# An attention, expert and dense block in one program: routing inside the attention block, and expert tiles gathered row by row

## What is computed

```python
# 1: attention of 4 batches x 8 heads, 576 positions, head size 64
scores = scale * q_rot @ k_rot.T ;  attn = softmax(scores) ;  x = attn @ v      # -> [2304, 512]
# 2: one expert of eight for each token
logits = (x / (|x| + 1e-6)) @ (emb / (|emb| + 1e-6)).T / tau
e = argmax(logits) ;  gate = softmax(logits)[e]
y = gate * (relu(x @ w1[e]) @ w2[e])                                          # 512 -> 1024 -> 512
# 3: dense
h = y @ w_in ;  out = (h - tanh(h)) @ w_out                                   # 512 -> 2048 -> 512
```

## Time and profile before

| | us |
|---|---|
| median of 3 runs (lowest, highest) | 1116.12 (1115.24, 1118.18) |
| the profiled execution's own time | 1110.96 |
| its span in the trace | 1109.1 |
| PE busy / DVE / ACT / POOL | 985.1 / 595.5 / 582.4 / 415.7 |
| mean granted clock of TensorE | 0.964 |

### The profile page before, as it was taken

How to read it: one execution, slowest core, us unless ns; L and a number is a source line. 1 busy time by engine, 2 the same in 40 slices (tenths; PEclk the granted TensorE clock), 3 DMA queues, 4 the chain that set the end, 5 groups by cost and what they waited for, 6 DMA issues and landing times. The chain is left out here.

```text
span 1109.1 us, 18954 instructions
## 1 busy us (share of the span) xinstructions
PE 985.1 (89%) x5604; PEld 871.1 (79%) x5605; DVE 595.5 (54%) x1195; ACT 582.4 (53%) x1273; POOL 415.7 (37%) x246
## 2 busy tenths in 40 slices
PE   1899999999995039999999976999999999999996
PEld 1899899989984038888888855888989889899895
DVE  4677777777773731111111104777666666666764
ACT  1677777777772632222322214666565565655653
POOL 3998788887510428309948305000000000000000
PEclk9999999999998569999999997999999999999999
DMA  8777777767503455314433106111000000000001
GB/s 236 192 207 197 219 189 202 206 186 205 145 21 90 169 188 202 97 47 151 152 123 113 38 30 200 58 48 48 1 19 10 0 28 0 13 15 0 28 2 28
DMA packets 63077, 113.82 MB, mean 103 GB/s; under 512 B 20032, under 2 KB 24640, under 8 KB 61120
## 3 DMA queue, kind: packets, MB, share of 16 engines
q1 hardware_dynamic: 52352, 92.62, 29.0%
q10 hardware_dynamic: 7808, 11.31, 3.2%
q0 software_dynamic: 2880, 9.44, 2.5%
HBM read 60.58 MB, written 24.41 MB: 77 GB/s over the span
## 5 line engine op out<-in xcount | busy, mean ns | idle before, releaser
L1429 PE MATMUL hd_ps<-y_hi,w_hi 128*128 128x384 f32 x384 | 130.9, 341 | 7.8 <-DVE g_sb L1599 7.8
L1429 PE MATMUL hd_ps<-y_lo,w_hi 128*128 128x384 f32 x384 | 129.6, 338 | 0.0
L1429 PE MATMUL hd_ps<-y_hi,w_lo 128*128 128x384 f32 x384 | 129.3, 337 | 0.0
L1499 ACT ACTIVATE mag<-hd_ps 128x384 f32<-128x384 f32 x96 | 47.3, 493 | 152.2 <-PE hd_ps L1429 149.8
L617 DVE TENSOR_REDUCE neg_max<-ps 128x1 f32<-128x576 f32 x144 | 108.1, 751 | 31.4 <-PE ps L373 28.9
L633 DVE TENSOR_TENSOR pt_lo<-ps,pt_hi 128x512 fp32r<-128x512 f32 x144 | 99.2, 690 | 43.3 <-ACT pt_hi L538 41.7
L538 ACT ACTIVATE pt_hi<-ps 128x512 fp32r<-128x512 f32 x144 | 86.8, 604 | 58.9 <-PE ps L420 57.5
L1447 PE MATMUL o_ps<-w_hi,g_hi 128*128 128x512 f32 x288 | 115.0, 399 | 2.2 <-DVE g_lo L1608 2.2
L1447 PE MATMUL o_ps<-w_hi,g_lo 128*128 128x512 f32 x288 | 114.3, 397 | 0.0
L1608 DVE TENSOR_TENSOR g_lo<-g_sb,g_hi 128x384 fp32r<-128x384 f32 x96 | 53.5, 558 | 112.3 <-ACT g_hi L1514 112.3
L1447 PE MATMUL o_ps<-w_lo,g_hi 128*128 128x512 f32 x288 | 113.5, 394 | 0.0
(11 more groups left out here) (208 smaller groups left out, 2429.8 us busy)
## 6 DMA issues: line engine op xcount, KB each, us to landing
w_stage<-in_w SPq DMA_DIRECT2D x32, 512.0 KB, 3.6
raw_qk<-in_qk SPq DMA_DIRECT2D x14, 1152.0 KB, 6.1
k_hh<-qk_hi SPq DMA_DIRECT2D x64, 144.0 KB, 2.8
k_ll<-qk_lo SPq DMA_DIRECT2D x64, 144.0 KB, 2.9
sorted_rows<-zeros SPq DMA_DIRECT2D x28, 256.0 KB, 6.2
x_row<-sorted_rows ACTq DMA_DIRECT2D x20, 256.0 KB, 2.7
y_rows<-y_row ACTq DMA_DIRECT2D x20, 256.0 KB, 2.1
q_st<-qk_hi SPq DMA_DIRECT2D x32, 144.0 KB, 3.0
```

The lines of the kernel that those rows point to most:

```text
L1429: op = nc.tensor.matmul(hd_ps[f % 2][:, 0:G], w[:, c, cols], y[:, c, :], start=c == 0 and h == 0, stop=c == DC - 1 and h == 2)
```

## The change

**One block less.** `routing` is gone; its work stands at the end of each engine's part of `attention`. All buffers of attention are laid by hand (`spots`) over the place where the weights will be, so that the first weights can be split before the block ends.

**A normalised table, first thing.** The router table is squared, summed, square-rooted and inverted before the first rotation, and multiplied by 1/(norm tau) into `fold_sb`. The logits' shares then come out of the fold matmul ready.

**A gather in place of the scatter.** Token rows are stored in token order in `x_rows` (SP, plain DMAs, three of four batches during pair 12). From the slots a table of token numbers `gid` is made: `slot_hot` (which slot in a tile) times `tile_ids` (token number, for the tile it lies in), 18 matmuls with 50 columns. Tile t is then gathered by an indirect DMA with `gid[:, t]`. The first gather is issued in `attention`, seven at the start of `experts`, 17 after the first weight set split by POOL.

**Around it.** Three of the 18 square sums go into pair 14 on ACT, the other 15 behind the last pair. Slots and plan use scans and bit masks. `gate` is computed inside `experts`. The first half of the first expert's weights is rounded by ACT in `attention` (L832 there), its low half split in `experts`, and the tile 0 `up` does the products with the low weights last. PE's tile loop is written out: 15 tiles straight, 7 each under an If. The 28 clears of `sorted_rows` and two of three loads of the identity matrix are gone.

```diff
 def attention(...)                                     # tensor engine, behind the last fold
+            pe.wait_ge(hot_done, 1)
+            nc.tensor.matmul(total_ps, sums_r[:, 1, :], hot[:, 6:8 + E * T], start=True, stop=True).then_inc(counted, 1)
+            nc.tensor.matmul(rank_ps..., sums_r[:, 0, :], hot[:, 8:8 + E * T], start=True, stop=True).then_inc(ranked, 1)
+            for t in range(T):
+                if t % (T // 3) == 0:
+                    pe.wait_ge(slots_hot, t // (T // 3) + 1)
+                last = nc.tensor.matmul(id_ps, slot_hot[:, t, :], tile_ids[:, t, :, :]..., start=t == 0, stop=t == T - 1)
+            last.then_inc(ids_ready, 1)
...
 # vector engine, ahead of rope_first
+            dve.wait_ge(emb_in, 32)
+            nc.vector.tensor_tensor(emb_sq[:], emb_sb[:], emb_sb[:], ALU.mult).then_inc(emb_squared, 1)
+            dve.wait_ge(emb_summed, 1)
+            nc.vector.tensor_scalar(emb_n[:, 0, :], norm_ps, 1e-30, None, ALU.max).then_inc(emb_clamped, 1)
+            dve.wait_ge(emb_root, 1)
+            newton(chain, nc, emb_n[:, 2, :], emb_n[:, 1, :], emb_n[:, 0, :], emb_n[:, 3, :])
+            chain(nc.vector.tensor_scalar(emb_n[:, 4, :], emb_n[:, 2, :], inv_tau, None, ALU.mult))
             dve.wait_ge(tables_in, 32)
             rope_first(1, first_k_in, first_k_mult, first_k_done)
...
 # sync engine
-                if clears:
-                    for i in range(2):
-                        clear(sorted_dram, p * 2 - 2 + i)
+            body(PAIRS - 4, 0, more_raw=False)
+            for b in range(B - 1):
+                store_main(b, slice(0, D))
+            for t in range(T, MT):
+                sp.dma_start(y_dram[t * P:(t + 1) * P, :], zeros[:]).then_inc(zeroed, 16)
+            body(PAIRS - 3, 1, more_raw=False)
...
+            sp.wait_ge(x_done, PAIRS * 2)
+            pass_tail(PAIRS - 1, 1, "logits", last_logits)
+            store_main(B - 1, late)
+            pass_tail(PAIRS - 1, 1, "rows", last_in)
+            sp.wait_ge(first_set, 1)
+            for c in range(UP):
+                sp.dma_start(staged(stage, c), weight_chunk(a["w1"], a["w2"], expert, c)).then_inc(w_in0[c], 16)
...
 # gpsimd
-            pool.wait_ge(pos_done, 1)
-            for t in range(T):
-                pool.indirect_dma_start(sorted_dram, bass.IndirectOffsetOnAxis(pos_i[:, t:t + 1], 0),
-                                        x_all[:, t, :], None).then_inc(scattered, 16)
+            pool.wait_ge(gid_done, 1)
+            gather_x(nc, x_dram, rows, gid, 0).then_inc(first_x, 16)
...
 # experts: tensor and scalar engine
-            with pe.Fori(1, MT - 2) as t:
-                with pe.If(t < fourth + 2):
+            for t in range(1, T - 2):
+                tile(t)
+            for t in range(T - 2, MT - 2):
+                with pe.If(fourth > t - 2):
                     tile(t)
...
+            nc.scalar.activation(work[:], work[:], ACT.Exp).then_inc(exp_done, 1)
+            tile(0, start=True, split=True)
```

More of the change, by code:

```diff
@@ L68, in attention @@
         MAIN = FULL * P
[L70 to L88, removed]
@@ L490, in body @@
                         values(p, r, follow[i][1])
+            pe.wait_ge(sums_set, 1)
+            pe.wait_ge(emb_squared, 1)
+            for c in range(DC):
+                last = nc.tensor.matmul(norm_ps, sums[:, 1, :], emb_sq[:, c, :], start=c == 0, stop=c == DC - 1)
+            last.then_inc(emb_summed, 1)
             pe.wait_ge(cleared, 1)
@@ L598, in _ @@
+            act.wait_ge(last_in, 32)
+            square(T - 1)
+            act.wait_ge(first_set, 1)
+            slot = act.value_load(plan[0:1, SLOT, 0:1], min_val=0, max_val=1)
+            for c in range(UP):
+                act.wait_ge(w_in0[c], 16)
+                nc.scalar.activation(chunk_of(w_hi, slot, c), stage[:, c, :], ACT.Identity).then_inc(w_hi0, 1)
+            act.wait_ge(sq_done, T)
+            nc.scalar.activation(norm[:, 1, :], norm[:, 0, :], ACT.Sqrt, bias=least)
         @block.vector
@@ L766, in routing @@
-        logits = sb("logits", [P, T, E])
-        work = sb("work", [P, T, E])
-        onehot = sb("onehot", [P, T, E])
-        col = sb("col", [P, 4, T])
-        scan = [sb(f"scan{r}", [P, PAD + T, E]) for r in range(2)]
-        base = sb("base", [P, T, E])
-        over = sb("over", [P, E, T])
-        escan = [sb(f"escan{r}", [P, EPAD + E]) for r in range(2)]
-        start = sb("start", [P, E])
-        first_row = sb("first_row", [P, E])
-        parity = sb("parity", [P, E])
-        has = sb("has", [P, 4, E])
@@ L1115, in _, with gather @@
                     split_set(before, slot)
+            def gather(t):
+                if t >= HELD:
+                    pool.wait_ge(xt_ready, t - HELD + 1)
+                gather_x(nc, x_dram, rows, gid, t).then_inc(x_in[t], 16)
+            nc.gpsimd.memset(one[:], 1.0).then_inc(one_set, 1)
+            for t in range(1, AHEAD):
+                gather(t)
+            pool.wait_ge(one_set, 1)
+            pool.wait_ge(w_split, CHUNKS)
+            last = pool.value_load(plan[0:1, LAST, 0:1], min_val=0, max_val=E - 1)
+            with pool.Fori(0, 1) as before:
+                next_set(before)
+            for t in range(AHEAD, MT):
+                gather(t)
+            with pool.Fori(1, E - 1) as before:
+                next_set(before)
             split_set(last, 0)
+            for t in range(1, MT):
+                pool.wait_ge(x_in[t], 16)
         @block.tensor
```

804 lines of the change are left out of this document (451 added, 353 removed).

## The result

| | before | changed kernel |
|---|---|---|
| median of the runs, us | 1116.5 (4 runs, 1115.24 to 1118.18) | 1106.51 (4 runs, 1106.22 to 1106.9) |
| profiled execution, us | 1110.96 | 1106.22 |
| its span, us | 1109.1 | 1104.4 |
| granted clock | 0.964 | 0.965 |

The ratio is 0.991, with a 95% interval of 0.9893 to 0.9927: 10.0 us gained where 23 were forecast. 1106.5 lies 2.5 above the range. The profile of the kernel before is an execution 5.5 faster than the median of its timed runs, so the two spans differ by less than the medians do.

What follows compares the result with a forecast made beforehand. PE was taken as nearly full except for a hole at the routing block and another at the start. Terms +5.2 + 1.0 - 31.6 + 2.5 = -22.9, from 1116.12, gave 1093 us; range 1086 to 1104.

Steps and rivals of the forecast that it cites:

- start: Beginning of the kernel: the first rope waits behind the router table's norm, delaying PE's first matmul, +5.2 us.
- last pairs: End of attention: three square sums added to ACT in pair 14 delay the exp that PE needs, +1.0 us.
- hole: Routing between attention and experts, PE nearly idle: the new chain brings the experts' first transpose earlier, -31.6 us.
- first tiles: Start of the experts: the second half of the weights is split later, so `down(0)` comes later, +2.5 us.
- Dense keeps its order: Dense stage after the experts: its order is unchanged, so the sum has no term for it.
- rival (b): PE's written-out tile loop: five skips over tiles' code cost 4.5 us, giving 1098; chance 0.08.
- POOL's 17 gathers ... = 21.6 us: Experts, behind POOL's first weight set: gathers of 1.27 us each, 21.6 us, hidden by POOL's 43.3 us of idle time.
- Rival (e): Experts: gathers of 4.2 us each on POOL delay the second weight set by 33 us, giving 1126; chance 0.05.
- rival (d): Late attention: stores and clears ahead of SP's last stacking make pair 15 wait about 9 us, 1102; chance 0.06.
- rival (a): Routing: the index chain is dearer, 3.1 us for strided reads and about 2 for scans and int32, 1098; chance 0.16.
- the 5.2: Whole kernel: the median of the runs is 5.2 us above the profiled execution, 1110.96; the forecast starts from that median.

Runs made afterwards that it cites:

- e5: The changed kernel, unchanged, run again on a chip where the kernel before takes 1111.15 us: 1090.16 us, ratio 0.9809.
- e2: Changed kernel with only PE's seven conditional tiles in a run-time loop, VectorE copying their rows to one fixed place: 1083.69 us, ratio 0.9761.
- e4: The kernel before with only PE's tile loop written out, 15 tiles straight and 7 each under an If: 1119.56 us, ratio 1.0076.
- e14: Changed kernel with the 17 gathers split, eight behind the first weight set and nine behind the second: 1096.73 us, ratio 0.9825.
- e21: Changed kernel with all 24 gathers ahead of the first weight set, on a chip with stalls: 1105.84 us, ratio 0.9917.
- e6: Changed kernel with VectorE roping first and doing the table's norm behind `by_cos` and `by_sin`: 1092.8 us, ratio 0.9828.
- e9: Changed kernel with ScalarE's queue issuing the cosine and sine tables ahead of the expert table and tau: 1109.79 us.
- e10: Changed kernel with the cosine and sine tables first in ScalarE's queue and the ropes ahead of the norm on VectorE: 1106.16 us.
- e15: The kernel before, unchanged, run for its trace on a further chip: 1111.59 us, one execution.
- e11: Changed kernel with late tiles in a run-time loop (rows staged from tile 18 on), tables and ropes first, gates' exp early: 1098.21 us, ratio 0.9818.
- e12: Changed kernel with the exp of the gates, with its table load, moved ahead of `take_x(1)`: 1109.54 us.
- e20: Changed kernel with late tiles in a run-time loop, start reordered, exp before the first relu, gathers in two parts: 1087.08 us, ratio 0.9744.
- e1: Changed kernel with all PE tiles in a run-time loop, VectorE copying each tile's rows to one fixed place: 1084.89 us, ratio 0.9772.

## Why the prediction was wrong

On chip A 10.0 us were gained, 12.9 less than forecast. Of these, 16.4 are what the changed kernel loses between chip C and chip A (1090.16 and 1106.51), less 5.4 that the kernel before loses between them (1111.15 and 1116.5), and 1.9 are missing on chip C too. On a quiet chip the forecast was nearly right: 22.9 forecast, 21.0 measured by the medians (e5), 20.8 by the spans. Term by term, from e5's trace against before's:

| term | forecast | e5 | how |
|---|---|---|---|
| start | +5.2 | +5.0 | first matmul 27.37 against 22.33 |
| last pairs | +1.0 | 0.0 | first matmul to last `x_done`: 325.28 against 325.30 |
| hole | -31.6 | -32.0 | 22.44 against 54.46 |
| first tiles | +2.5 | +2.5 | `down(0)` 21.34 against 18.84 |
| the rest | 0 | +3.7 | 691.9 from `down(0)` to the end, against 688.2 |

- **The step that failed first: "Dense keeps its order" and the sum without a term for TensorE's new code.** The rival (b) named the place and the mechanism (five skips, TensorE's code fetched) and priced it at 4.5 with a chance of 0.08. The wait grew by 5.5 (6.37 against 0.90), 2.3 more went at the lower clock behind it, and the skips cost 7.6 against a loop (e2), 7.2 in the kernel before (e4). The argument against it, that the empty rounds of the run-time loop fit into 0.9, said nothing on written-out skips. This was partly paid by 3.7 that the rest of the tile loop gained (249.19 with the loop against 252.88 before): a full tile takes 12.51 in before and in e4, and 12.35 in the changed kernel, with a loop or without, 2.7 for 16 tiles. No experiment shows why.
- **The step that failed most: "POOL's 17 gathers ... = 21.6 us" hidden.** They were, for GpSimd: 0.95 each at a pitch of 1.25, as forecast (1.27), and no weight set came late. Rival (e) looked only at GpSimd's queue. On chip A the other engines stopped beside them: from `down(0)` to dense 268.7 against 256.8 in e5 (11.9), in dense 440.0 against 435.1 (4.9). Together 16.8; at `down(0)` the trace of chip A was 0.7 ahead of e5's, so 16.1 of span, and 16.4 between the medians. That the stall in the tile loop goes with the gathers is shown by two kernels: split in two groups, it nearly goes (e14, 8.7 back); moved, it moves (e21). For the 4.9 in dense no experiment moved the gathers. Why a run of gathers does this on some chips and not on others is open. Their form (a matmul per 1.4 to 2.1 us with nothing to wait for, three engines at once) fits late instructions; that is argued, no row shows a fetch that waits.
- **Start: right number, half the cause.** By e5's trace two more issues in ScalarE's queue cost 2.5, not 1.1 (table load at 10.93, was 8.40), so the square root came at 12.23 in place of 10.9 and the first rope at 13.82 in place of 12.5. The last copy then landed 2.3 after its issue in place of 4.4; I had taken 0.7 for that, 1.4 at the most, and it was 2.1. The two errors cancel, which is luck. And the chain was not the only hold: the tables behind two small loads were another (e6, e9, e10). A change in the order of a queue has to be read for what moved back, not only for what moved forward.
- **Last pairs: 1.0 too much.** The three squares of pair 14 lay wholly in ScalarE's idle time, as did the stores of rival (d) in the queues.
- **First tiles: the right number, in part by luck.** TensorE's granted clock is 0.50 from the first transpose on, after the hole in which it stood nearly idle. It rose after 6 us in before's trace and in chip A's, where `down(0)` came 18.84 and 20.14 behind the transpose, and after 8 us in e15, e4 and e5, where it came after 19.92, 20.05 and 21.34. Like with like, the change cost 1.3 to 1.4 here, not 2.5; the rest of e5's +2.5 is the clock of that execution. The same stretch in before's trace and in e15's (the clock third from the right):

```profile
408.09:410.09 2.00, 2.00 (x10) 1.58 (x9) 1.69 (x2) 0.86 (x2) 0.00 (x0) 0.94 0.16 61
```

```profile
408.25:410.25 2.00, 2.00 (x6) 1.52 (x6) 1.77 (x2) 1.25 (x2) 0.00 (x0) 0.50 0.16 59
```

- **Hole: right within 0.4**, in its parts too (by chip A's trace): SP's two issues and landing 2.5 (forecast 2.5), `gid` 17.6 behind `x_done` (17.4), plan's end at 375.00, 21.9 behind it (22.3). So rival (a) didn't come.
- **The range** took its lower and upper ends from mechanisms inside the kernel. Nothing in it stood for a kernel that takes 1111 on one chip or in one execution and 1116.5 in another, though before's own profile (1110.96) and timed runs (1116.12) differed by just that. I added the 5.2 as a constant. It was a sign that something in the kernel is sensitive to where or when it runs, and the change added more of it (5.4 before, 16.4 after).

## What to carry to other kernels

Where a profile and the timed runs of the same kernel differ by much more than the runs among themselves, ask what differs before adding it as a constant: here it was a sensitivity that the change tripled. On some chips a long row of indirect transfers went with stalls of engines that have nothing to do with them; spread them over the work in groups, and look for waits without a releaser on all engines at once. Compare such a wait with the usual one at the same place, and price a stall by the time from one tile to the next. Steps that may be skipped did better in a run-time loop; steps that always run could be written out at no cost. When loads are put at the head of a queue, list what now lands later, and keep small VectorE operations out of the time in which GpSimd works on wide tiles.

## What the runs showed of the hardware that I had not expected

- The same kernel in six places (chips A to F): before 1110.9 and 1111.2 on two, 1114.6 to 1116.9 on four. The changed kernel 1090.2 on one of the first kind, 1105.5 and 1106.5 on two of the second. On the second kind single executions are fast too (1109.24 for before on D). What sets a chip or an execution apart stays open, and so does what before loses there.
- On the second kind, TensorE, ScalarE and VectorE stand at once while indirect gathers are issued or have just been: with 17 in a row ScalarE's wait is 14.4 to 16.0 in one piece in five traces (chips A, D and E) and in two or three pieces in two more (e11, e12), and one tile of TensorE takes 10.6 to 12.1 more. Eight behind the first set cost TensorE nothing, nine behind the second 1.5 in e14 and 2.1 in e20. ScalarE and VectorE run their tiles as loops and stand all the same, so written-out code is not needed for it. Whether TensorE in a full loop (e1) is spared wasn't tried on such a chip.
- Behind five skipped tiles of written-out code TensorE waits 5.7 to 6.6 in one piece (eleven traces; in e4 4.9 in three), and then works at half clock for some 4.6 us; the same five rounds of a loop cost 0.9.
- A VectorE operation on 8 columns took 2.19 to 2.60 beside a GpSimd operation on 1152, and 0.17 to 0.23 without it.
